# GpSimd's leak in pairs of tiles and over four groups, and a tile-by-tile wait ahead of the second weight product

## What is computed

```python
scores = scale * q @ k.T
kth = np.partition(scores, -32, axis=-1)[..., -32:-31]
attn = softmax(where(scores >= kth, scores, -1e9))
x = attn @ v                                  # 2304 tokens x 512
h = x @ w_in                                  # 2304 x 2048
g = np.maximum(h, 0.0) + alpha * np.minimum(h, 0.0)
x2 = g @ w_out                                # 2304 x 512
out = x2 + gate * (relu(x2 @ w1[e]) @ w2[e])  # for tokens that aren't skipped
```

## Time and profile before

| | |
|---|---|
| median of 3 executions | 1143.64 us (1143.39 to 1148.92) |
| the profiled execution | 1143.76 us, of which its instructions span 1142.0 us |
| TensorE busy (matmuls) | 929.2 us, 81% |
| VectorE busy | 913.3 us, 80% |
| ScalarE busy | 624.2 us, 55% |
| GpSimd busy | 430.4 us, 38% |

### The profile page before, as it was taken

One profiled execution on the slowest core, in us unless ns is written; L12 is line 12 of the kernel. 1 busy time (PEld: TensorE's weight loads), 2 busy tenths in 40 slices (PEclk: granted clock), 3 DMA queues, 4 the chain that ended last, 5 costly groups with the idle time before them and its releaser, 6 DMA issues.

```text
span 1142.0 us, 22616 instructions
## 1 busy us (share of the span) xinstructions
PE 929.2 (81%) x6288; PEld 621.1 (54%) x6289; DVE 913.3 (80%) x2061; ACT 624.2 (55%) x1291; POOL 430.4 (38%) x597
## 2 busy tenths in 40 slices
PE   5235578898899889888988898899888887499896
PEld 3123346575667557665766575666657565244343
DVE  4899979999999999999999999999999252311111
ACT  3775949637854784587469647845873461011010
POOL 0145637612841582167038514830681100101010
PEclk9666679999999999999999999999999899599899
DMA  7910201004001300310031013002000366444640
GB/s 210 354 32 3 50 22 33 22 2 118 7 21 53 73 0 21 92 34 21 1 102 23 21 34 91 0 21 73 23 1 1 116 222 226 139 162 142 219 145 18
DMA packets 98660, 84.08 MB, mean 74 GB/s; under 512 B 69116, under 2 KB 77308, under 8 KB 98048
## 3 DMA queue, kind: packets, MB, share of 16 engines
q1 hardware_dynamic: 94544, 78.56, 22.6%
q0 software_dynamic: 1488, 3.15, 0.8%
q10 hardware_dynamic: 2528, 1.18, 0.4%
HBM read 72.64 MB, written 11.53 MB: 74 GB/s over the span
## 4 chain that ended last, share of the span: by engine, by line
PE 57%; issue 10%; ACT 10%; POOL 10%; DVE 6%; DMA 4%; SPq 1%; POOLq 1%; ACTq 0%; DVEq 0%
PE acc L583 16%; PE acc L552 7%; PE sc L523 6%; PE acc L570 5%; PE pt_full L541 4%; POOL pos_part L347 4%; PE sc L687 3%; POOL arena L349 2%; PE pt_full L754 2%; ACT arena L821 2%; PE pt_full L762 2%; POOL arena L1317 2%; DMA arena<-in_moe_w_dram 2%; PE acc L592 2%; DVE best L1032 1%
## 5 line engine op out<-in xcount | busy, mean ns | idle before, releaser
L1032 DVE MAX8 best<-arena 128x8 f32<-128x576 f32 x576 | 403.5, 741 | 9.6 <-ACT arena L814 9.6
L1045 DVE MATCH_REPLACE8 arena<-best,arena 128x576 f32<-128x576 f32 x432 | 315.7, 738 | 0.0
L1317 POOL TENSOR_SCALAR arena<-arena,row_inv 128x576 f32<-128x576 f32 x144 | 106.1, 753 | 365.7 <-DVE row_inv L1065 365.7
L570 PE MATMUL acc<-arena 128*128 (+1 forms) x1536 | 202.5, 286 | 24.6 <-ACT neg_part L860 22.7
L583 PE MATMUL acc<-arena 128*128 128x288 f16 x1536 | 200.9, 288 | 2.9 <-DVE arena L351 2.9
L570 PEld LDWEIGHTS acc<-arena 128*128 128x128 f16 x1536 | 146.3, 98 | 75.5 <-issue 33.9
L583 PEld LDWEIGHTS acc<-arena 128*128 128x128 f16 x1536 | 148.9, 98 | 48.9 <-issue 9.7
L541 PE MATMUL pt_full<-ident,arena 128*128 128x128 f32 x576 | 99.7, 301 | 76.8 <-POOL arena L1317 36.1
L814 ACT ACTIVATE arena<-sc 128x576 f32<-128x576 f32 x144 | 92.1, 642 | 85.9 <-PE sc L523 69.5
L1053 DVE SCALAR_TENSOR_TENSOR arena<-arena,best 128x576 f32<-128x576 f32 x144 | 128.6, 940 | 6.4 <-ACT arena L821 6.4
L541 PEld LDWEIGHTS pt_full<-ident,arena 128*128 128x128 f32 x576 | 71.3, 152 | 106.7 <-issue 61.8
(11 more groups left out here) (170 smaller groups left out, 1025.1 us busy)
## 6 DMA issues: line engine op xcount, KB each, us to landing
arena<-in_moe_w_dram SPq DMA_DIRECT2D x64, 512.0 KB
nat<-in_v_dram SPq DMA_DIRECT2D x64, 128.0 KB, 2.2
nat<-in_k_dram SPq DMA_DIRECT2D x60, 128.0 KB, 2.8
x_rows<-x2n SPq DMA_DIRECT2D x24, 192.0 KB, 2.4
out_dram<-x2n SPq DMA_DIRECT2D x24, 192.0 KB, 2.6
nat<-in_q_dram SPq DMA_DIRECT2D x64, 64.0 KB, 2.1
arena<-in_moe_w_in_dram SPq DMA_DIRECT2D x4, 1024.0 KB, 7.4
arena<-in_moe_w_out_dram SPq DMA_DIRECT2D x4, 1024.0 KB, 13.3
```

What stands on the lines that cost most here:

```text
L570: last = nc.tensor.matmul(dst[:, 0:HALF], win16[:, a, d, f * P:(f + 1) * P], xT16[:, bass.ds(row + d, 1), b, :].rearrange("p b s -> p (b s)"),
L1032: nc.vector.max(best[:, gp, j, r, :], src).then_inc(max_found if r == 0 else dve_step, 1)
L1045: nc.vector.match_replace(left[:, j, :], best[:, gp, j, r, :], src, MASKED).then_inc(dve_step, 1)
L1317: nc.gpsimd.tensor_scalar(probs[:, gp, j, :], probs[:, gp, j, :], row_inv[:, gp, j:j + 1], 1.0, ALU.mult, ALU.mult)\
```

## The change

`leak` gets an argument `at_once`. With 2, it runs the adds of two tiles, then both roundings, then both subtractions, so that each step of a tile has the other tile's step between itself and the next. Only GpSimd uses 2, VectorE after the loop keeps 1. GpSimd's tiles are dealt out anew: 0 to 4 behind the normalise of (0, 0), 5 to 9 behind (0, 1), 10 to 14 behind (0, 2), and 15 behind (1, 0). The wait of `down` for all 16 tiles is replaced, in its first quarter (d = 0), by a wait for each tile ahead of its three matmuls. The arithmetic is the same.

```diff
-        def leak(engine, unit, m, fs):
-
-            for f in fs:
-                n = LEAK_STEPS * (FT1 * m + f)
-                pos, neg = pos_part[:, f % NEG, :], neg_part[:, f % NEG, :]
-                hold(engine, parts_ready, FT1 * m + f + 1)
-                unit.tensor_tensor(pos, pos, neg, ALU.add).then_inc(leak_ready, 1)
-                hold(engine, leak_ready, n + 1)
-                unit.tensor_scalar(gT16[0][:, f, :], pos, 1.0, 1.0, ALU.mult, ALU.mult).then_inc(leak_ready, 1)
-                hold(engine, leak_ready, n + 2)
-                unit.tensor_tensor(gT16[1][:, f, :], pos, gT16[0][:, f, :], ALU.subtract).then_inc(g_ready, 1)
+        def leak(engine, unit, m, fs, at_once=1):
+
+            for first in range(0, len(fs), at_once):
+                some = fs[first:first + at_once]
+                n = LEAK_STEPS * (FT1 * m + some[0])
+                for i, f in enumerate(some):
+                    hold(engine, parts_ready, FT1 * m + f + 1)
+                    unit.tensor_tensor(pos_part[:, f % NEG, :], pos_part[:, f % NEG, :], neg_part[:, f % NEG, :], ALU.add).then_inc(leak_ready, 1)
+                for i, f in enumerate(some):
+                    hold(engine, leak_ready, n + i + 1)
+                    unit.tensor_scalar(gT16[0][:, f, :], pos_part[:, f % NEG, :], 1.0, 1.0, ALU.mult, ALU.mult).then_inc(leak_ready, 1)
+                for i, f in enumerate(some):
+                    hold(engine, leak_ready, n + len(some) + i + 1)
+                    unit.tensor_tensor(gT16[1][:, f, :], pos_part[:, f % NEG, :], gT16[0][:, f, :], ALU.subtract).then_inc(g_ready, 1)
...
             def down(m, items, d, fs):
 
                 if fs[0] == 0:
-                    if d == 0:
-                        hold(pe, g_ready, NEG + FT1 * (m + 1))
                     items.open = begin(items)
                 for f in fs:
+                    if d == 0:
+                        hold(pe, g_ready, NEG + FT1 * m + f + 1)
                     for n, (a, b) in enumerate(PASSES):
...
-            leak_parts = {(0, 0): range(0, 5), (0, 1): range(5, 12), (0, 2): range(12, FT1)}
+            leak_parts = {(0, 0): range(0, 5), (0, 1): range(5, 10), (0, 2): range(10, 15), (1, 0): range(15, FT1)}
...
-                        leak(pool, nc.gpsimd, i - MLP_LAG, leak_parts.get((par, g), ()))
+                        leak(pool, nc.gpsimd, i - MLP_LAG, leak_parts.get((par, g), ()), 2)
```

## The result

The changed kernel took **1184.36 us** (median of 4, 1179.72 to 1195.52) against 1146.28 us of the kernel before, run beside it: a ratio of **1.0346, 95% interval 1.0297 to 1.0395**. The forecast was 1139.5 us with a range of 1132 to 1149. The kernel is slower, and by far more than any rival allowed.

A forecast was written before the change was run, and what follows sets the result against it. Two loops of nearly one length bound the kernel: VectorE's, full at 104.94 of 106 us, and one through GpSimd, TensorE and ScalarE. 1143.6 - 4.4 (end) + 0.3 (loop) = 1139.5 us, range 1132 to 1149.

The forecast's parts named there:

- The end: After the loop, the down product starts right behind the up product: 2.88 us of wait plus 1.56 of clock, 4.4 gained.
- Register waits at zero: Fifteen more waits a pass on TensorE's queue in the loop's down product, taken as costing zero; farther bound 2.4 us.
- Two at a time: GpSimd's leak in pairs: two tiles in about 3.74 us, normalise (0,1) 0.7 us earlier a pass.
- Tile 10: Leaked behind normalise (0,2), done 5.24 us after it; ScalarE's tile 14 waits, first transpose store at 21.3 instead of 20.57: +0.7.
- the way from that store to the exponentials: In group (1,0), from ScalarE's first transpose store to the exponentials, taken as 4.8 us; L1053 0.93 us later.
- the clock fall in two passes of seven: TensorE idles 1.4 to 3 us before the next transpose; clock falls cost 2 x 1.4 us, loop sum +0.3.
- GpSimd's loop, -0.35 us a pass: Loop over GpSimd: -0.7 from pairs, +0.7 from tile 10, -0.35 from TensorE's work done ahead, a pass.
- VectorE's loop shrink to 105.5: VectorE's loop: L1053 0.93 us later, but port free and L1062 saves 0.45, so about 105.5 us a pass.
- Tile 15: In the loop, leaked behind normalise (1,0), ready at 542 us; the down product needs it after 544, so nothing waits.
- The third: Rival: gap behind tile 14 cools TensorE every pass, 1.05 us each, 1146.6 us, or 1153 with later exponentials; chance 0.22.
- The register waits show: Rival: 15 x 0.16 = 2.4 us a pass on TensorE, less 0.35, seven times, less 4.4: 1153.6 us; chance 0.06.
- a period above 107: Sign of being wrong: loop passes above 107 us, where L552 to L552 was expected between 105.4 and 106.9.

The follow-up runs named there:

- t1: The kernel before with only the sixteen tile-by-tile waits of the down product, in the loop and after it, GpSimd unchanged: 1147.52 us, 0.999 of before.
- u3: The whole change with all sixteen waits in the loop, but tile 10 back behind (0,1), parts 5, 6, 4, 1: 1167.56 us, 1.0214 of before.
- w2: The kernel before with tile-by-tile waits, each of the sixteen standing three times, GpSimd's order unchanged: 1176.7 us, 1.0226 of before.
- t4: The whole change, but the loop's down product waits twice (fifteen tiles, then the last) instead of sixteen times: 1170.73 us, 1.0213 of before.
- t5: GpSimd pairs in the parts of before (5, 7, 4), one wait in the loop, tile waits at the end only: 1146.54 us, 1.0022 of before.
- u1: The whole change with two waits in the loop and tile 10 back behind (0,1), parts 5, 6, 4, 1: 1158.63 us, 1.011 of before.
- t8: Pairs that pause before rounding and subtraction, parts of before (5, 7, 4), one wait in the loop, tile waits at the end: 1157.64 us, 1.0132 of before.

## Why the prediction was wrong, and where it was right

*The end.* Right: 4.6 us against 4.4 in the trace, 3.05 of it from the gap and the rest from the clock (the down product takes 23.68 us). The timed runs show 0.26 and 0.2 per cent, some 2 to 3 us; the second interval still holds no change. This is all of the change that is worth having, and no kernel here beats before by more.

*Register waits at zero.* Right for what I priced, the bubble (t1: 0.999; in the change L586 idles 0.0 us). Wrong as a whole: the step looked at the time of a wait on its engine and never at the length of the loop in instructions. The missing term is a fetch in two of six passes. With u3's and w2's passes with and without, it is 6 to 9 us for each, so by my estimate 12 to 18 us of the change; t4 against the change says 1.3 per cent, 15 us.

*Two at a time.* The pair takes 3.70 us (643.23 to 646.93), as counted (3.74). The 0.7 us that I booked as gained shows nowhere: t5 is 1.0022. With the pauses gone VectorE gets in later: beside a leak the rows had a masking instruction at 1.27 and 1.34 us, and at the head of (0,2) it now takes 1.49 to 2.92 us, where it took 0.79 to 0.85 before. The prediction had no term for that. The runs with pauses show that this is not what makes the time.

*Tile 10.* The chain was right link by link: L862 5.25 us behind the normalise (5.24 forecast), the store 2.71 later (2.97), the normalise 0.32 us behind its inverse, the three L1056 of (1,0) at 0.8 us. **The term that failed is the way from that store to the exponentials: 6.88 us where I took 4.8.** I let the clock fall in two passes of seven and at 1.4 us each. It fell in every pass behind this gap (3.08 to 3.30 us of idle, just above my 1.4 to 3), it stayed low into the weighted sum (7.04 us instead of 5.54), for which the prediction had no term, and the exponential, forecast 0.93 us late, is 2.42.

*The second failure is what a late exponential is worth.* I balanced it against GpSimd's loop, -0.35 us a pass, and let VectorE's loop shrink to 105.5 by the port waits saved. Apart from its wait the search of (1,0) did get 1.1 us shorter in the pass accounted above, but those of (0,1) and (0,2) got 0.3 and 0.6 us longer beside trains without a pause, so nearly nothing was left to pay with. VectorE, busy 104.94 of 106 us, passed every wait on in full: 2.42 + 1.40 gave 3.8. And the delay came round a second time, at (0,0), half a pass later, through the slow weighted sum, in some passes with a fall of the clock at (0,0) as well. The prediction had no row on that place.

*Tile 15.* "Nothing waits" was right for TensorE, and still the tile costs: u1 against t5, 1.011 against 1.0022. The runs put it behind the fall of the clock at (0,0) in u1, and don't say what triggers that.

*The rivals.* The third had the mechanism and the sign, with 1.05 us a pass and 1146.6 to 1153 us; passes without a fetch cost 2.2 to 6.7 us, 4.8 on average. "The register waits show" had the right culprit for the wrong reason. The mark named as wrong, a period above 107, is what came. The Trainium skill's rule on gaps between groups of matmuls (TensorE: Matmul & The Clock Gate, HAM oscillation), weighed as a rival, pointed the right way here: the granted clock is 0.926 over the profiled execution before and 0.878 over that after (0.913 to 0.943 and 0.878 to 0.908 over all that were timed).

| step | forecast, us | measured, us |
|---|---|---|
| end of the kernel | -4.4 | -4.6 |
| pairing | -0.7 a pass, in GpSimd's loop | none to be told (t5) |
| store to exponentials at (1,0) | 4.8 | 6.88 |
| wait of L1056 at (1,0) | 0.93 | 2.42 |
| wait of L1056 at (0,0), no fetch | none | 0 to 3.88 |
| pass without a fetch | 105.4 to 106.9 | 108.1 to 112.6 |
| pass with a fetch | not foreseen | 118.9, 119.3 |
| loop | +0.3 (seven passes) | +44.5 (six passes) |

## What to carry to other kernels

When one engine fills 99 per cent of a pass, cost every edit by what arrives late at that engine, at each place where it waits for another, and not by the loop that the chain happens to name. A short wait moved in front of an in-order queue takes all behind it along, and if TensorE idles meanwhile, the clock multiplies the delay. Before adding instructions to a long loop, count those it has and look at whether its instruction queue moves in the loop: what costs nothing by itself (t1) brought fetches beside GpSimd's new order (the change, u3) or three times over (w2).

## What the runs showed of the hardware

- A loop of TensorE of 720 matmuls and 902 other records may or may not be fetched again at its branch: none in t1, two passes of six in the change, and with 934 four of six. The branch then lasts 3.4 to 5.6 us instead of 0.22, nine blocks of 16 KB follow over some 100 us, and the clock is at 0.51 to 0.76 for the first 21 us (after, u3, u4, w2).
- TensorE's clock fell behind an idle time of 3.08 to 3.30 us in front of the second transposes of (0,2) in all seven passes of the change, where before it idled 0.99 us ahead of the first ones, and the clock stayed at 1.00 (523.6 to 530). In the one of 671 us four fp32 transposes took 1.08 us instead of 0.60, and the weighted sum 6.89 us instead of 5.5.
- An instruction of VectorE with two SBUF inputs (0.80 us alone) took 2.85 us in three passes of seven beside a GpSimd train with no pause, and ended 0.45 us after the train's first pause, of 0.16 us, was over. The Trainium skill (SBUF — State Buffer, Who interferes with whom) has the one block the other for a whole instruction; here VectorE was passed over by several: at 649.19 one rounding, two subtractions and an add went by at their usual lengths.
- Profiled executions needn't stand for the median: t8's had a span of 1141.5 us, its runs a median of 1157.64.
